# Attention set step by step between the matmul groups of two gated convolutions, on one core

## The chip, the cores and the metric

The kernel runs on one core of a Trainium2 chip. The metric is the time of one execution on the device, in microseconds (us). The time before is 488.39 us, the median of 3 runs (485.01 to 489.94).

## The reference

Three computations in a row. B = 4, H = 8 heads of 64 columns, S = 576, so the model width is 512.

```python
scores = (q @ k.T) / 8 + slope[h] * -abs(i - j)      # where 0 <= i - j < 128, else -1e9
attn = exp(scores - max(scores)); attn /= sum(attn) + 1e-9
x = attn @ v                                          # heads side by side: (4, 576, 512)

h = relu(x @ w_in)                                    # 1024 wide
g = h * sigmoid(conv3(h, taps1))                      # 3 taps along the sequence
x2 = g @ w_out                                        # 512 wide

gate = sigmoid(conv5(x2, taps2))                      # 5 taps, looking back
y = (gate * (x2 @ w_val)) @ w_out2
```

All is float32. The four weight products are made in three matmuls each, of tensors split in two parts (`hi` is the value rounded to fp32r, `lo` what is left): hi*hi, hi*lo, lo*hi.

## The kernel before, in words

Each engine has a program of its own, in a fixed order, and semaphores between them. There are two phases.

**Attention.** A step is one tile of 128 queries of one pair of heads: 4 batches x 4 pairs x 5 tiles = 80 steps; the fifth tile has 64 queries. Per step: TensorE makes the scores (`scores`, L743, a float32 matmul is two instructions in the trace, matmuls at L756); VectorE adds the bias and takes the maximum (`scores`, L567, L582); ScalarE makes the exp and its sum (`exps`, L401, L408); VectorE adds 1e-9 (`guard`, L596), inverts (`invert`, L605) and scales (`normalise`, L614); TensorE transposes (`turn`, L760, L777); ScalarE, for the fifth tile VectorE, copies the transposes out (`copy_out`, L422 and L626); TensorE multiplies by v (`mix`, L780, L805 and L808); ScalarE copies the result to `x_all` (`x_rows`, L430 and L433). The order is pair by pair, all five tiles of a pair. Scores run 5 steps ahead (`AHEAD`), with 5 buffers of probs, 2 banks each for scores, transposes and outputs. Meanwhile SyncE loads 12 weight panels (128 x 1024) into two raw buffers, one behind each pair's q and k, and GpSimd splits each: a cast to `w_hi` (L345) and a subtraction to `w_lo` (L348).

**Gated convolutions.** 8 chunks of 288 rows of the sequence, one half of a batch each. TensorE's order in a chunk c (`chunk`, L910): `up(c)` (8 groups of 12 matmuls of 290 columns), `val(c-1)` (4 groups), `down(c)` (4 groups of 24), `out(c-1)` (4 groups): 288 matmuls, all at L839 to L841 (in chunk 0 the first `down` is at L893 to L895). VectorE makes the taps of one block in the first convolution (`tap_rows`, L668 and L672), woven so that tap 0 of the next block stands between taps 1 and 2 of this one; then `gated` (L680), `val_rows` (L690), and five taps of the second convolution (`conv2_rows`, L702 and L706). ScalarE copies out of the banks, makes the sigmoids (L470, L493) and the `hi` parts (L479, L488, L511, and L450 for x), GpSimd the `lo` parts (L370, L362, L379, and L356 for x). `val_rows(0)` stands between the last two `gated`.

The loops over batches and chunks are loops on the engines (`Fori`).

Of the kernel before, what the change touches and what calls it, by code (L numbers as in the profile page):

```python
# [13 lines left out]
P = 128  # L14

# [5 lines left out]
SUBS = SEQ // SUB  # L25
SEEN = WINDOW + SUB
STEPS = PAIRS * TILES


AHEAD = 5  # L30
RING = TILES
SCALE = HEAD ** -0.5
MASKED = -1e9
# [3 lines left out]
EARLY = 16  # L37
# [27 lines left out]
def attention_and_gated_convolutions(nc, q_in, k_in, v_in, panels_in, taps1_in, taps2_in, y_out):  # L65
    with ExitStack() as ctx:
# [6 lines left out]


# [9 lines left out]

        w_hi = place("w_hi", [P, PANELS, PANEL], F32R)
        w_lo = place("w_lo", [P, PANELS, PANEL], F32R)
        x_all = place("x_all", [P, BATCH * PAIRS * SEQ])
        x_hi = place("x_hi", [P, KM, READ], F32R)
        x_lo = place("x_lo", [P, KM, READ], F32R)
        taps1 = place("taps1", [P, TAPS1, KW])  # L90
        taps2 = place("taps2", [P, TAPS2, KM])
        shared = top[0]


        q_heads = [place(f"q_heads{s}", [P, SUBS, 2, SUB]) for s in range(2)]
        k_pair = [place(f"k_pair{s}", [P, SEQ]) for s in range(2)]
        v_pair = [place(f"v_pair{s}", [P, TILES, P]) for s in range(2)]
        bias = place("bias", [P, PAIRS, SEEN])
        distance = place("distance", [P, SEEN])
# [7 lines left out]
        w_raw = [place(f"w_raw{r}", [P, PANEL]) for r in range(2)]  # L107


        top[0] = shared  # L110
        g1_hi = place("g1_hi", [P, KW, HALF], F32R)
        g1_lo = place("g1_lo", [P, KW, HALF], F32R)
        x2_all = place("x2_all", [P, KM, LEFT + SEQ])
# [7 lines left out]
        g2 = [place(f"g2_{r}", [P, HALF]) for r in range(2)]  # L121
        y_sb = [place(f"y_sb{r}", [P, HALF]) for r in range(2)]


        banks = [psum(f"bank{n}", [P, 512]) for n in range(8)]
        s_ps = [banks[0], banks[1]]
        t_ps = [banks[2], banks[3]]
        o_ps = [banks[4], banks[5]]
        o_tail_ps = banks[6]


        h_ps = x2_ps = banks[0:4]
# [829 lines left out]
```

## Time and profile before

| | before |
|---|---|
| median of 3 runs | 488.39 us |
| lowest and highest | 485.01, 489.94 us |
| profiled execution, span | 489.8 us |
| profiled execution, listed time nearest to the span | 489.94 us |
| instructions | 10856 |

The profile is one execution. PE is TensorE's matmuls, PEld its weight loads, DVE is VectorE, ACT is ScalarE, POOL is GpSimd, SP is SyncE, which issues the DMAs. The span goes from the first to the last instruction. Matmuls are pipelined, so a matmul's duration is longer than the time from one to the next. PEclk is the granted TensorE clock, 1.00 being 2.4 GHz and 0.50 being 1.2 GHz.

### The profile page before, as it was taken

The page shows a single profiled execution, that of the slowest core. Times are in us where ns is not written, and L with a number is a line of the kernel's source. Part 1 is how long each engine was busy: PE and PEld are TensorE (multiplying, and loading weights), DVE is VectorE, ACT ScalarE, POOL GpSimd, SP SyncE. Part 2 cuts the span into 40 slices and gives each one's busy share as a digit, 9 for nine tenths or more (in the row PEclk, how much of TensorE's full clock was granted, in tenths as well). Part 3 has the DMA queues.
Part 4 walks back from the last instruction along what each step waited for, and adds up shares of the span by engine and source line. Part 5 has one row for each costly group of instructions (what it writes and reads, how often), then busy time and mean ns, then how long its engine had stood idle before and what let it go on. Part 6 is the DMA issues. An engine that isn't in the chain of part 4 may idle for free.

```text
span 489.8 us, 10856 instructions
## 1 busy us (share of the span) xinstructions
PE 453.4 (93%) x3424; PEld 415.2 (85%) x3424; DVE 370.8 (76%) x1078; ACT 247.8 (51%) x746; POOL 177.9 (36%) x181
## 2 busy tenths in 40 slices
PE   4989788887889998999999999999999999999997
PEld 3767566665667897998999999999999999999996
DVE  5889967787767586896696786977968769669750
ACT  3777656775748563354354355255344344435432
POOL 2223522243310026157148136326425605713611
PEclk9999979998879998999999999999999999999999
DMA  5465435433413000000100000010010010010011
GB/s 146 116 176 149 148 106 168 154 115 115 141 49 98 1 2 0 2 1 1 50 1 1 32 17 0 12 36 0 0 48 0 0 48 0 0 48 2 1 48 50
DMA packets 37626, 25.52 MB, mean 52 GB/s; under 512 B 20704, under 2 KB 34016, under 8 KB 37600
## 3 DMA queue, kind: packets, MB, share of 16 engines
q1 hardware_dynamic: 37600, 25.20, 17.1%
q8 instruction: 14, 0.23, 0.2%
q14 instruction: 12, 0.10, 0.1%
HBM read 20.47 MB, written 4.72 MB: 51 GB/s over the span
## 4 chain that ended last, share of the span: by engine, by line
issue 33%; PE 28%; DVE 17%; POOL 16%; ACT 2%; DMA 1%; POOLq 1%; DVEq 0%; SPq 0%; ACTq 0%; PEldq 0%
POOL g_lo L370 10%; PE bank L756 7%; PE bank L777 7%; PE bank L808 5%; DVE guarded L596 4%; POOL x_lo L379 4%; DVE probs L614 3%; DVE conv L672 3%; PE bank L839 2%; PE bank L841 2%; PE bank L840 2%; POOL g_lo L362 2%; DVE gate L706 2%; DVE conv L680 1%; DVE probs L582 1%
## 5 line engine op out<-in xcount | busy, mean ns | idle before, releaser
L839 PE MATMUL bank<-x_hi,w_hi 128*128 128x290 f32 (+1 forms) x384 | 113.8, 296 | 0.5 <-ACT hidden L464 0.5
L840 PE MATMUL bank<-x_lo,w_hi 128*128 128x290 f32 (+1 forms) x384 | 113.7, 296 | 0.0
L841 PE MATMUL bank<-x_hi,w_lo 128*128 128x290 f32 (+1 forms) x384 | 113.7, 296 | 0.0
L839 PE MATMUL bank<-g_hi,w_hi 128*128 128x288 f32 x352 | 105.4, 300 | 3.2 <-POOL g_lo L370 1.7
L370 POOL TENSOR_TENSOR g_lo<-conv,g_hi 128x288 fp32r<-128x288 f32 x64 | 60.2, 949 | 131.2 <-ACT g_hi L479 131.2
L840 PE MATMUL bank<-g_lo,w_hi 128*128 128x288 f32 x352 | 103.9, 295 | 0.0
L841 PE MATMUL bank<-g_hi,w_lo 128*128 128x288 f32 x352 | 103.6, 294 | 0.0
L706 DVE SCALAR_TENSOR_TENSOR gate<-x_all,taps,gate 128x288 f32<-128x288 f32 x128 | 80.7, 630 | 4.5
L672 DVE SCALAR_TENSOR_TENSOR conv<-hidden,taps,conv 128x288 f32<-128x288 f32 x128 | 83.4, 657 | 0.6
L839 PEld LDWEIGHTS bank<-x_hi,w_hi 128*128 128x128 f32 x384 | 72.3, 188 | 0.8 <-ACT hidden L464 0.8
L840 PEld LDWEIGHTS bank<-x_lo,w_hi 128*128 128x128 f32 x384 | 72.8, 189 | 0.0
L841 PEld LDWEIGHTS bank<-x_hi,w_lo 128*128 128x128 f32 x384 | 72.5, 189 | 0.0
L408 ACT ACTIVATE probs<-probs,neg_max 128x192 f32<-128x192 f32 (+1 forms) x144 | 62.1, 434 | 20.2 <-DVE neg_max L582 19.2
L839 PEld LDWEIGHTS bank<-g_hi,w_hi 128*128 128x128 f32 x352 | 66.1, 188 | 6.8 <-POOL g_lo L370 5.7
L582 DVE CUSTOM_DVE_ANT_0 probs<-bank,bias 128x192 f32<-128x192 f32 (+1 forms) x144 | 46.5, 324 | 31.3 <-PE bank L756 22.0
L756 PE MATMUL bank<-k_pair,q_heads 128*128 128x192 f32 (+2 forms) x288 | 63.3, 345 | 6.9 <-DMA k_pair<-k_t 6.9
L777 PE MATMUL bank<-identity,probs 128*128 128x128 f32 x256 | 48.8, 306 | 20.4 <-DVE probs L614 20.2
L841 PEld LDWEIGHTS bank<-g_hi,w_lo 128*128 128x128 f32 x352 | 66.2, 188 | 0.0
L840 PEld LDWEIGHTS bank<-g_lo,w_hi 128*128 128x128 f32 x352 | 66.1, 188 | 0.0
L777 PEld LDWEIGHTS bank<-identity,probs 128*128 128x128 f32 x256 | 28.5, 149 | 35.2 <-DVE probs L614 24.1
L470 ACT ACTIVATE conv<-conv 128x288 f32<-128x288 f32 x64 | 28.5, 445 | 54.8 <-DVE conv L672 54.8
L756 PEld LDWEIGHTS bank<-k_pair,q_heads 128*128 128x128 f32 x288 | 49.4, 214 | 7.0 <-issue 6.8
(55 smaller groups left out, 670.8 us busy)
## 6 DMA issues: line engine op xcount, KB each, us to landing
w_raw<-panels SPq DMA_DIRECT2D x12, 512.0 KB, 4.2
q_heads<-q_t SPq DMA_DIRECT2D x32, 144.0 KB, 3.1
k_pair<-k_t SPq DMA_DIRECT2D x16, 288.0 KB, 3.7
y_t<-y_sb SPq DMA_DIRECT2D x32, 144.0 KB, 1.8
v_pair<-v_pairs SPq DMA_DIRECT2D x16, 256.0 KB, 2.7
v_pair<-v_pairs SPq DMA_DIRECT2D x16, 32.0 KB, 2.5
taps<-taps SPq DMA_DIRECT2D x1, 12.0 KB, 3.6
taps<-taps SPq DMA_DIRECT2D x1, 10.0 KB, 3.9
```

What stands on the lines that cost most here:

```text
L370: pool.tensor_tensor(g1_lo[:, m, :], conv[m % DEPTH][:, :], g1_hi[:, m, :], ALU.subtract).then_inc(g1_lo_done, 1)
L408: last = act.activation(probs[r][:, half, lo:hi], probs[r][:, half, lo:hi], ACT.Exp, bias=neg_max[r][:, half:half + 1], scale=-1.0, accum_ ...
L470: act.activation(conv[m % DEPTH][:, :], conv[m % DEPTH][:, :], ACT.Sigmoid).then_inc(gate1_done, 1)
L582: last = dve.tensor_tensor_reduce(probs[r][:, half, lo:hi], s[:, 2 * P * half + lo:2 * P * half + hi], bias_of(hp, t, half), -SCALE, 3e38, ...
L672: dve.scalar_tensor_tensor(out=out, in0=rows, scalar=taps1[:, tap, m:m + 1], in1=out, op0=ALU.mult, op1=ALU.add).then_inc(tap1_done if tap ...
L706: dve.scalar_tensor_tensor(out=out, in0=x2_all[:, m, at + tap:at + tap + HALF], scalar=taps2[:, tap, m:m + 1], in1=out, op0=ALU.mult, op1= ...
L756: last = pe.matmul(s[:, 2 * P * half + lo:2 * P * half + hi], q[:, 2 * t + half, :, :], k[:, first_key + lo:first_key + hi], start=True, s ...
L777: last = pe.transpose(out[:, at:at + P], p[:, half, col:col + P], identity[:, :])
L808: last = pe.matmul(o_ps[hp % 2][rows, t * P:(t + 1) * P], v[:, key_tile, rows], turned_probs, start=(j == 0), stop=(j == blocks - 1))
L839: pe.matmul(out, w_hi[:, p, col:col + P], hi[k], start=first, stop=False)
L840: pe.matmul(out, w_hi[:, p, col:col + P], lo[k], start=False, stop=False)
L841: last = pe.matmul(out, w_lo[:, p, col:col + P], hi[k], start=False, stop=final)
```

## The change

The program of each engine is written out in full over 9 x 24 beats, without loops. A beat of TensorE is one group of 12 matmuls. The attention steps go tile by tile over the four pairs of heads. Steps 0 to 11 (three tiles) run alone at the start; the others are set singly between beats: in even chunks c the steps 12 to 19 of the same batch before the beats 12 to 19 (`down`), in chunks 1, 3 and 5 the steps 0 to 11 of the next batch before the beats 10 to 21. Around each such beat TensorE runs `turn(step)` and `scores(step + 3)` before it and `mix(step)` behind it. Sigmoids stand in the beats 0 to 8.

Scores run 3 ahead with 4 buffers of probs; there is one bank for transposes and one for outputs, `mix` of a tile's first step waiting for `x_lo_done` of the tile before. x is no longer kept in float32: ScalarE casts the output bank to `x_hi` and VectorE subtracts to `x_lo`, per tile. Weight panels are loaded into the memory of `w_lo` and split in place; GpSimd splits six of them before the walk and six in chunk 0. All `copy_out` are ScalarE's. `hidden` and `conv` have 3 buffers instead of 4. The taps of a block are no longer woven with the next block's. q, k and v are laid out by tile on the host. Core of the diff:

```diff
-AHEAD = 5
-RING = TILES
+LOOK = 3
+RING = LOOK + 1
+V_RING = 3
+BEATS = 24
+VAL0, DOWN0, OUT0 = KW, KW + KM, BEATS - KM
-DEPTH = 4
+DEPTH = 3
...
+        def steps_before(c, j):
+            if c % 2 == 0 and c < CHUNKS and 0 <= j - DOWN0 < 8:
+                return [STEPS * (c // 2) + 12 + j - DOWN0]
+            if c % 2 == 1 and c < CHUNKS - 1 and 0 <= j - DOWN0 + 2 < 12:
+                return [STEPS * (c // 2 + 1) + j - DOWN0 + 2]
+            return []
+        def walk(slot, close, beat):
+            for step in range(12):
+                slot(step)
+                if step:
+                    close(step - 1)
+            close(11)
+            for c in range(CHUNKS + 1):
+                for j in range(BEATS):
+                    for step in steps_before(c, j):
+                        slot(step)
+                    beat(c, j)
+                    for step in steps_before(c, j):
+                        close(step)
...
# SyncE
+            load_queries_and_keys(0)
+            load_values(0)
+            load_panel(0)
+            load_queries_and_keys(1)
+            load_values(1)
+            sp.dma_start(taps1[:, :, :], taps1_in).then_inc(taps_loaded, 16)
+            sp.dma_start(taps2[:, :, :], taps2_in).then_inc(taps_loaded, 16)
+            load_panel(1)
+            load_panel(2)
...
# GpSimd
+            def beat(c, j):
+                if c < CHUNKS and 2 <= j < KW + 2:
+                    g1_low(c, j - 2)
+                if c > 0 and 0 <= j - VAL0 - 2 < KM:
+                    g2_low(c - 1, j - VAL0 - 2)
+                if c < CHUNKS and j == VAL0 + 3:
+                    keep_history(c)
+                if c < CHUNKS and j >= DOWN0 + 2 and j < DOWN0 + 2 + 2 * KM and j % 2 == 0:
+                    x2_low(c, (j - DOWN0 - 2) // 2)
+                if c == 0:
+                    for n in {3: (6,), 6: (7,), 14: (8, 9), 18: (10, 11)}.get(j, ()):
+                        split_panel(n)
+            for n in range(6):
+                split_panel(n)
+            walk(slot, slot, beat)
...
# ScalarE
+            def slot(step):
+                _, t, _ = where(step)
+                cols = 2 * P if t in (0, FULL) else 4 * P
+                act.wait_ge(turned, step + 1)
+                reach(act, mixed, step - 1)
+                act.copy(probs_t[step % 2][:, 0:cols], t_ps[:, 0:cols]).then_inc(copied, 1)
+                if step + LOOK - 1 < ALL_STEPS:
+                    exps(step + LOOK - 1)
...
+            def beat(c, j):
+                if c < CHUNKS and j < KW:
+                    hidden_rows(c, j)
+                if c < CHUNKS and 1 <= j < KW + 1:
+                    gate_rows(c, j - 1)
+                if c > 0 and j < KM:
+                    gate2_rows(c - 1, j)
+                if c < CHUNKS and 2 <= j < KW + 2:
+                    g1_high(c, j - 2)
+                if c > 0 and 0 <= j - VAL0 - 1 < KM:
+                    g2_high(c - 1, j - VAL0 - 1)
+                if c < CHUNKS and DOWN0 <= j < OUT0 and j % 2 == 1:
+                    x2_rows(c, (j - DOWN0) // 2)
+                if c > 0 and j >= OUT0:
+                    out_rows(c - 1, j - OUT0)
...
# VectorE
+            def slot(step):
+                if step + 1 < ALL_STEPS:
+                    normalise(step + 1)
+                if step + LOOK < ALL_STEPS:
+                    scores(step + LOOK)
...
+            def beat(c, j):
+                if c < CHUNKS and j < KW:
+                    tap_rows(c, j)
+                if c < CHUNKS and 1 <= j < KW + 1:
+                    gated(c, j - 1)
+                if c > 0 and 0 <= j - VAL0 < KM:
+                    val_rows(c - 1, j - VAL0)
+                if c < CHUNKS and DOWN0 + 2 <= j <= OUT0 and j % 2 == 0:
+                    conv2_rows(c, (j - DOWN0 - 2) // 2)
...
+            dve.wait_ge(taps_loaded, 32)
+            normalise(0)
+            walk(slot, close, beat)
...
# TensorE
+            def slot(step):
+                turn(step)
+                if step + LOOK < ALL_STEPS:
+                    scores(step + LOOK)
...
+            def beat(c, j):
+                if c < CHUNKS and j < VAL0:
+                    up(c, j)
+                if c > 0 and VAL0 <= j < DOWN0:
+                    val(c - 1, j - VAL0)
+                if c < CHUNKS and DOWN0 <= j < OUT0:
+                    down(c, (j - DOWN0) // 2, (j - DOWN0) % 2)
+                if c > 0 and j >= OUT0:
+                    out(c - 1, j - OUT0)
...
+            walk(slot, mix, beat)
```

`down(c, m, 0)` now waits for `g2_done` of the chunk before (its bank is the one `val` wrote), `out(c, 0)` for all four `g2_lo` of its chunk, `up(c, m)` for `y_kept` of the chunk c-2, and `up(c, 0)` for `x_lo_done` of the tiles it reads. On ScalarE and VectorE `close` of the last pair's step makes `x_hi` and `x_lo`; VectorE's `normalise` is now guard, invert and the two scalings in a row, each waiting for the one before.

## Rows read from the trace of the kernel before

**Rows 1.** The page: busy time of each engine, share of the span, instructions
```profile
PE 453.4 (93%) x3424; PEld 415.2 (85%) x3424; DVE 370.8 (76%) x1078; ACT 247.8 (51%) x746; POOL 177.9 (36%) x181
```
**Rows 2.** Stretches: its length, busy us (instructions) of each engine, clock, DMA share, GB/s
```profile
12.10:166.30 154.20, 134.02 (x1096) 101.46 (x1096) 121.34 (x591) 104.64 (x373) 43.49 (x25) 0.93 0.41 122
...
238.70:278.00 39.30, 39.16 (x293) 38.70 (x292) 30.89 (x58) 17.21 (x45) 16.99 (x17) 1.00 0.05 16
```
**Rows 3.** Timeline of TensorE, attention and both ends: start, us, what [idle before]
```profile
12.10 0.66 PE L777 MATMUL bank<-identity,probs 128*128 128x128 f32 x2 [0.22 <-DVE probs L614]
...
34.75 0.66 PE L777 MATMUL bank<-identity,probs 128*128 128x128 f32 x4 [1.22 <-DVE probs L614]
...
137.00 1.11 PE L777 MATMUL bank<-identity,probs 128*128 128x128 f32 x4 [3.48 <-DVE probs L614]
...
146.23 0.65 PE L777 MATMUL bank<-identity,probs 128*128 128x128 f32 x4
...
154.12 0.65 PE L777 MATMUL bank<-identity,probs 128*128 128x128 f32 x4
...
166.88 0.40 PE L839 MATMUL bank<-x_hi,w_hi 128*128 128x290 f32 x1
...
486.65 0.29 PE L841 MATMUL bank<-g_hi,w_lo 128*128 128x288 f32 x1
```
**Rows 4.** Timeline of TensorE in one chunk: first `up` and first `down` matmul
```profile
238.69 0.30 PE L839 MATMUL bank<-x_hi,w_hi 128*128 128x290 f32 x1
...
257.92 0.30 PE L839 MATMUL bank<-g_hi,w_hi 128*128 128x288 f32 x1
```
**Rows 5.** Timeline around one panel's split; then an undisturbed round of five steps
```profile
30.20 1.04 POOL L345 CAST w_hi<-w_raw 128x1024 f32 x1 [5.65 <-DMA w_raw<-panels]
...
30.38 1.20 DVE L614 TENSOR_SCALAR probs<-probs,inverse 128x192 f32<-128x192 f32 x2
...
31.41 2.39 POOL L348 TENSOR_TENSOR w_lo<-w_raw,w_hi 128x1024 f32 x1 [0.17 <-POOL w_hi L345]
31.51 2.32 DVE L596 TENSOR_SCALAR guarded<-total 128x2 f32<-128x2 f32 x1
...
34.16 0.54 DVE L614 TENSOR_SCALAR probs<-probs,inverse 128x192 f32<-128x192 f32 x2
...
146.23:154.12 7.89, 7.89 (x73) 6.05 (x71) 6.05 (x40) 6.59 (x26) 0.00 (x0) 1.00 0.42 112
```
**Rows 6.** The stretch behind the idle time that ends at 137.00
```profile
137.00:143.00 6.00, 6.00 (x28) 4.79 (x30) 2.02 (x17) 2.77 (x10) 0.00 (x0) 0.51 0.02 6
```
**Rows 7.** DMA issues: count, size of one, median us from issue to landing
```profile
w_raw<-panels SPq DMA_DIRECT2D x12, 512.0 KB, 4.2
```
**Rows 8.** Timeline of VectorE in the chunks
```profile
237.83 2.18 DVE L706 SCALAR_TENSOR_TENSOR gate<-x_all,taps,gate 128x288 f32<-128x288 f32 x4
...
250.03 0.51 DVE L672 SCALAR_TENSOR_TENSOR conv<-hidden,taps,conv 128x288 f32<-128x288 f32 x1
250.46 0.45 DVE L680 TENSOR_TENSOR conv<-hidden,conv 128x288 f32<-128x288 f32 x1
250.83 0.51 DVE L672 SCALAR_TENSOR_TENSOR conv<-hidden,taps,conv 128x288 f32<-128x288 f32 x1
...
251.54 1.06 DVE L672 SCALAR_TENSOR_TENSOR conv<-hidden,taps,conv 128x288 f32<-128x288 f32 x1
...
253.60 1.06 DVE L672 SCALAR_TENSOR_TENSOR conv<-hidden,taps,conv 128x288 f32<-128x288 f32 x1
...
270.58 0.36 DVE L702 TENSOR_SCALAR gate<-x_all,taps 128x288 f32<-128x288 f32 x1
...
273.50 0.37 DVE L702 TENSOR_SCALAR gate<-x_all,taps 128x288 f32<-128x288 f32 x1
```
**Rows 9.** Timeline of ScalarE: the first Sigmoid
```profile
172.45 1.28 ACT L470 ACT_TABLE_LOAD   x1
173.75 0.45 ACT L470 ACTIVATE conv<-conv 128x288 f32<-128x288 f32 x1
```

More of the change, by code:

```diff
@@ L453, in _ @@
-            for t in range(AHEAD - 1):
-                exps(0, 0, t)
-            copy_out(0, 0, 0)
-            batches(act, batch_tiles, lambda: split_x(0, 0, 0))
+            def slot(step):
+                _, t, _ = where(step)
+                cols = 2 * P if t in (0, FULL) else 4 * P
[4 more added lines that the diff above has]
+                    exps(step + LOOK - 1)
@@ L711, in chunk @@
[L711 to L729 removed]
+            for step in range(LOOK):
+                scores(step)
@@ L758, in scores, with turn @@
                 last.then_inc(scores_done, 1)
[L760 to L771 removed]
+            def turn(step):
+                _, t, _ = where(step)
+                pe.wait_ge(probs_normal, step + 1)
+                reach(pe, copied, step)
@@ L811, in mix @@
-                last.then_inc(mixed, 1)
-            def batch_tiles(b, last):
-                for hp in range(PAIRS):
-                    for t in range(TILES):
-                        ahead(b, hp, t, last, 1, turn)
-                        ahead(b, hp, t, last, AHEAD, scores)
-                        mix(b, hp, t)
+                        last = pe.matmul(o_ps[rows, P * hp:P * hp + SUB * subs],
+                                         v_tile[key_tile % V_RING][0:keys, P * hp + HEAD * h:P * hp + HEAD * (h + 1)],
+                                         turned_probs[0:keys, :, j, h, :], start=(j == 0),
+                                         stop=(j == blocks - 1))
@@ new lines, in mix, with slot, product @@
+                last.then_inc(mixed, 1)
+            def slot(step):
+                turn(step)
+                if step + LOOK < ALL_STEPS:
+                    scores(step + LOOK)
+            def product(out, w_at, hi, lo, of, first=True, final=True):
+                for i, k in enumerate(of):
+                    p, col = w_at(k)
+                    start, stop = first and i == 0, final and i == len(of) - 1
+                    pe.matmul(out, w_hi[:, p, col:col + P], hi(k), start=start, stop=False)
+                    pe.matmul(out, w_hi[:, p, col:col + P], lo(k), start=False, stop=False)
+                    last = pe.matmul(out, w_lo[:, p, col:col + P], hi(k), start=False, stop=stop)
+                return last
@@ L900, in out @@
-            def out(c):
-                ready = lambda k: since(pe, g2_lo_done, KM * c + k + 1)
-                for m in range(KM):
-                    since(pe, g2_done, KM * c + m + 1)
-                    product(y_ps[m % KM][:, 0:HALF], lambda k: (P_OUT2 + k // 2, k % 2 * MODEL + m * P),
-                            rows_of(g2_hi, KM), rows_of(g2_lo, KM),
-                            None if m else ready).then_inc(y_done, 1)
-            def chunk(c, batch, half):
-                up(c)
-                if is_chunk(c, 0):
-                    first_down()
-                    return
-                val(c - 1)
-                down(c)
-                out(c - 1)
@@ L921, in _ @@
-            since(pe, w_split, PANELS)
-            chunks(pe, chunk)
-            val(CHUNKS - 1)
-            out(CHUNKS - 1)
+            walk(slot, mix, beat)
 def kernel(**inputs):
```

759 lines of the change are left out of this document (290 added, 469 removed).

## The prediction

> **What bounds the kernel now.** I read the page's busy shares first [rows 1]: TensorE is busy 453.4 of 489.8 us, far above every other engine, so the question is whether the change takes anything out of its idle time. Then the stretches [rows 2] and TensorE's timeline. Attention runs from the first transpose at 12.10 us to the first matmul of `up` at 166.88; the gated convolutions from there to the last matmul at 486.65, which ends at 486.9 [rows 3]; the last copy and store take the 2.9 up to 489.8. TensorE's clock in attention is 0.93 on average and 1.00 in the chunk of [rows 2]. The matmul rows give what TensorE needs without waits. Five attention steps in a row, undisturbed, take 154.12 - 146.23 = 7.89 us, 1.58 a step [rows 3]. From the first `up` to the first `down` of a chunk, 144 matmuls take 257.92 - 238.69 = 19.23 us, 0.1335 each [rows 4]; the chunks need 8 x 288 of them, 307.6 us. So TensorE's own need is 12.1 + 80 x 1.58 less 1.9 for three scores already made = 124.5, + 307.6 + 2.9 = 447. Before loses 43 us over that: some 30 in attention, 12.4 in the chunks. In steady state a chunk takes 39.3 us [rows 2], TensorE 38.4 of them. The most that the change can win is 43 us, and only by less waiting: no matmul goes away, so two things that are both TensorE's own work can't hide each other.
>
> Where do the 30 us of attention come from? Each panel's split on GpSimd is a cast of 1.04 and a subtraction of 2.39 us [rows 5]. VectorE's `normalise` beside the cast takes 1.20 us for two where 0.54 is normal, its `guard`, two columns wide, 2.32 beside the subtraction (it starts 0.10 after GpSimd's row and ends with it; I take 0.15 as its own). So one panel takes 0.7 + 2.2 = 2.9 us from VectorE, which is busy for only 6.05 us of a round's 7.89 [rows 5]; TensorE loses what is left over that slack, 1.22 us of idle in [rows 3]. And after the longer idle of 3.48 us before 137.00 its granted clock is 0.51 on average over 6 us, so at the lower of its two levels, 1.2 GHz of 2.4, for nearly all of them [rows 3, 6]: that loses 2.9. I argue from these two prices throughout: 2.9 us of VectorE a panel, and half speed after a long wait.
>
> **What is removed, added, moved.**
> Work that stays: all matmuls, exps, taps and splits. The Tensor program gets a fixed order: slot (turn, scores three steps on), one group of 12 matmuls, mix. Fewer buffers: one bank for transposes, one for the output, 4 rings for probs instead of 5, 3 for conv instead of 4. At the edges: `copy_out` of the last tile moves from VectorE to ScalarE (16 copies), x_lo from GpSimd to VectorE (20 times, 512 columns mostly; from the 0.45 of 288 columns [rows 8] I estimate 0.7 each, 14 us). TensorE's order doesn't feel these by themselves.
>
> Start. `normalise(0)` now waits for the taps, which are queued behind panel 0, q, k and v of tile 1. Before, the first transpose is at 12.10 [rows 3], with the same q and k ahead of it; a panel more in the queue is 4.2 us to landing [rows 7]. I let it stand at 12.1 (bounds 11 and 16).
>
> Prologue, 12 steps alone. TensorE needs 12 x 1.58 = 19.0 less the scores already made, so 17.0 and an end at 29.1. But six panels are now split in these first 30 us, where before GpSimd paused 5.65 us between two [rows 5]. Now it hardly pauses: a panel lands within 4.2 us [rows 7], 3.6 us of splitting follow, so about three are back to back. A step has three VectorE instructions that such a split stops (guard, two normalise) and a panel offers two boundaries, so while GpSimd works back to back I take one step per 3.5 us instead of 1.6 to 1.9. From 13 us: three panels, 11 us, 3 steps; then two more with gaps, 11 us, 4.5 steps; the other 4.5 steps at 1.9, 9 us; the first x tile's way bank, ScalarE, VectorE before the first `up` costs 2 us that no TensorE work covers. End: about 43. Bounds: 32 (VectorE's slack of 0.3 us a step takes up most of it) and 50. I take 43 since panel and step prices are rows. 14 us over need.
>
> Chunk 0. TensorE needs 192 x 0.1335 + 8 x 1.58 = 38.2. VectorE: a block of taps took 2.06 us in before's order (253.60 - 251.54), of which 0.55 is GpSimd's subtraction (the 1.06 where 0.51 is normal) [rows 8]. In the new order the three taps of a block follow each other, each waiting for the last; such a pair costs 0.55 (2.18 us for four, the last 0.51 long) where an unchained one costs 0.43 (250.46 - 250.03) and `gated` 0.37 (250.83 - 250.46) [rows 8]; tap 0 I take at 0.40. So 0.40 + 0.55 + 0.43 + 0.37 + 0.55 = 2.3 us a block, 18.4 for eight. A conv2 block is 2.92 us (273.50 - 270.58) [rows 8], four are 11.7. Attention steps: I take 6.05/5 = 1.21, plus 0.1 for chaining; eight are 10.5, two x tiles 1.4. Together 42, and now six panels on top, 6 x 2.9 = 17, of which the last 5 run on into the next chunk: 54, with some of it before and behind. Its first mix stands behind ScalarE's g1_high(7), which waits for all eight blocks and two panels, 25 us in, when TensorE is there at 16. I take 49 us (bounds 40 and 58), 11 over need.
>
> Chunks 1, 3, 5 (12 steps each). Need 288 x 0.1335 + 12 x 1.58 = 57.4. VectorE needs 18.4 + 4 x 0.4 + 12 x 1.31 + 3 x 0.7 + 11.7 = 49.5, so it isn't the bound of the sum. But it falls behind at the front: the taps start 2.4 us in (a group of 1.6, then copy and waits, estimated 0.8) and with the wait for the last sigmoid the last `gated` ends at 21.7; `val_rows(0)` and ScalarE's g1_high(7), g2_high(0) end at 22.6. ScalarE's queue holds the copy of the first interleaved step behind them: 23.2. TensorE wants that copy, for `mix` after beat 10, at 11 x 1.6 for the beats and 1.3 for one turn and scores (my share of 1.58 to 1.9), 18.9. Wait: 4.3 us. The low clock behind such a wait I price at 2.6 us, a little under the 2.9 of [rows 3, 6] (bounds 0, where a wait of 1.22 lowered nothing, and 2.9). 57.4 + 4.3 + 2.6 = 64.3, taken as 64.4. From there VectorE has 2.9 + 2 x 1.31 + 0.4 = 5.9 us of work for two beats of 2 x (1.6 + 1.58) = 6.4, so nothing further is lost. Chunk 1 takes over VectorE's lag from the late panels: 66.5.
>
> Chunks 2, 4, 6 (8 steps). Need 51.0. Here the slot comes before beat 12, `down`'s first part wants `g2_done` at 22.1 and TensorE is there at 12 x 1.6 + 1.2 = 20.4; the copy behind it is late by 0.3. 53.4. Chunk 7, without steps: there at 19.2, so 2.9 of wait and 0.7 of clock: 42.0, against 39.3 now: the early `val_rows(0)` and the taps woven into each other are what before saves. Tail: val and out 12.8, the chain from the last `val` to a now undivided wait for four g2_lo 2.1, end 2.9: 17.8.
>
> ScalarE: Exp and Sigmoid now alternate by chunk, 14 loads where there were two, 1.28 us each with the Sigmoid starting 1.30 after the load's start [rows 9]. ScalarE is busy 17.2 of 39.3 us [rows 2], so 14 x 1.28 = 18 us mostly fit in. The first exp of a set is needed two slots (6.8 us) later: cost nothing, up to 1.3 a set if the lag above eats it. The Trainium skill (ScalarE: Activation LUTs, What ACT_TABLE_LOAD costs) puts a switch at about 2.66 us, since a drain of 1.38 comes with it. Our row shows no such gap. By the page the loads would be 37 us of ScalarE; 1.4 more in each of 7 sets is the most that can reach TensorE, 10 us.
>
> The unrolled program is fetched instead of looped over; no row prices that, 0 to 5 us; I take 0.
>
> Sum: 43 + 49 + 66.5 + 2 x 64.4 + 3 x 53.4 + 42 + 17.8 = 507.3 against the span of 489.8. The listed time nearest this span is 489.94, so nothing lies around it; the median of the three is 488.39, 1.4 lower. Predicted: **506 us**.
>
> **Rivals.**
> (a) Faster. VectorE keeps step: if the eight tap blocks end by 18.9 us of a chunk (2.0 us a block rather than 2.3, gate and copy right behind), no wait at the first mix arises, and no low clock. Then chunks 1 to 7 lose nothing: 447 + 14 + 11 + 2 = 474. For it: before's own blocks take 2.06 [rows 8]. Against: three waits in a row per block and the in-order queue on ScalarE.
> (b) No change. The panels cost half: VectorE works between them, as in the round of [rows 3, 5] where a panel costs TensorE 1.22 us, and prologue and chunk 0 end at 36 and 43: 507 - 13 - 5 (no lag, less clock) = 489, 488 by the median.
> (c) Much slower. The slot's loop (copy, exp, normalise, turn, each behind another engine's queue) also stalls in each beat with conv2: 1 us for 16 such pairs and the clock at half more often: 525.
> (d) By the switch price of the drain: some 516. It asks for a gap of 1.4 us behind the table load, which the one row of a load amid work does not show.
>
> **How the numbers follow.** Forecast 0.55, (a) 0.13, (b) 0.12, (c) 0.14, (d) 0.06. The prologue's bounds alone are 32 and 50, chunk 0's 40 and 58. The range reaches into (a) and (c): 478 to 530. About 1% is what a measurement of this kernel can tell from no change. Faster by over 1% holds (a) and the low edge of the forecast, 0.15; within 1% (b), 0.13; slower the rest, 0.72.
>
> **What would show it.** Right: TensorE idle before the first `mix` of the odd chunks, 3 to 5 us, with ScalarE's copy of probs_t as what it waits for, and the clock at 0.5 behind it; the first `up` at 40 us or later; VectorE's guard and normalise at 2.3 us several times in the first 40 us; chunk 0 the only chunk with GpSimd busy over 30 us; 14 to 16 table loads. Wrong: a first `up` before 35, or chunks 3 and 5 under 60 us; a fall of TensorE's idle time below 30 us in all.

## The result, and the profile after

The changed kernel takes 512.43 us (median of 4 runs, 510.67 to 514.14), the kernel before 488.97 beside it: a ratio of 1.048, 95% interval 1.0415 to 1.0546. It is slower. The profiled execution took 511.86 us for a span of 509.9. The page of the changed kernel, busy time, and the chain that ended last by engine:

```profile
PE 453.4 (89%) x3424; PEld 421.6 (83%) x3424; DVE 382.4 (75%) x1080; ACT 259.9 (51%) x756; POOL 152.8 (30%) x178
...
PE 53%; DVE 33%; issue 6%; ACT 5%; SPq 1%; DMA 1%; POOLq 0%; POOL 0%; DVEq 0%
```

TensorE is busy for the same 453.4 us as in [rows 1], so the 20 us of added span show as TensorE's idle time. (The busy time holds what a lower clock costs; the mean clock is 0.956 here and 0.976 before.) The losses lie in few places. Stretches of the changed kernel from one first matmul of `up` to the next (columns as in [rows 2]): the 12 steps at the start, chunks 0 to 4, chunk 7, the tail.

```profile
13.80:45.35 31.55, 23.55 (x168) 17.79 (x169) 28.29 (x98) 17.97 (x63) 17.10 (x10) 0.95 0.58 188
45.35:106.98 61.63, 41.73 (x304) 38.40 (x304) 50.78 (x102) 24.26 (x68) 31.89 (x25) 0.83 0.14 41
106.98:172.04 65.06, 61.45 (x457) 57.32 (x457) 51.00 (x160) 36.17 (x108) 13.55 (x17) 0.95 0.12 34
172.04:222.84 50.80, 50.28 (x403) 47.38 (x401) 39.42 (x110) 28.11 (x80) 13.38 (x17) 1.00 0.15 42
222.84:287.11 64.27, 60.88 (x458) 56.48 (x457) 48.74 (x155) 36.57 (x109) 13.56 (x17) 0.95 0.16 43
287.11:337.90 50.79, 50.27 (x402) 47.36 (x401) 39.35 (x110) 28.12 (x80) 13.38 (x17) 1.00 0.15 41
450.82:490.62 39.80, 38.56 (x291) 38.33 (x289) 30.11 (x56) 17.60 (x45) 13.47 (x17) 1.00 0.05 16
490.62:509.90 19.28, 14.74 (x98) 14.27 (x96) 1.83 (x4) 5.07 (x13) 3.21 (x4) 0.90 0.13 45
```

Even chunks (172.04, 287.11) lose half a microsecond. The start loses 8 (31.55 less 23.55), chunk 0 loses 20 and ran at clock 0.83, odd chunks lose 3.5 and part of their clock. TensorE's waits by what ended them (total us, times, longest):

```profile
PE bank L621 <- DVE probs L512: 17.9, 14, 4.8
PE bank L642 <- ACT probs_t L387: 17.7, 4, 8.9
PE bank L658 <- DVE x_lo L527: 6.6, 2, 5.1
PE bank L607 <- DMA k_all<-k_t: 5.9, 1, 5.9
```

The first is `turn` waiting for `normalise`: 11.3 of it up to the first `up`, 4.8 of these before the first transpose, and 4.0 once in chunk 0. The second is the predicted wait: the first interleaved `mix` of chunks 0, 1, 3 and 5. Here is the one of chunk 3, 21.4 us into it, the timeline and then the clock (columns of a stretch as above):

```profile
243.37 0.43 ACT L427 CAST g_hi<-gate 128x288 fp32r<-128x288 f32 x1
243.71 0.37 ACT L387 COPY probs_t<-bank 128x256 f32<-128x256 f32 x1
244.09 1.28 ACT L376 ACT_TABLE_LOAD   x1
...
244.22 0.70 PE L642 MATMUL bank<-probs_t,v_tile 128*64 128x128 f32 x4 [2.96 <-ACT probs_t L387]
...
245.39 0.35 ACT L376 ACTIVATE probs<-probs,neg_max 128x64 f32<-128x64 f32 x1
```
```profile
245.00:247.00 2.00, 1.65 (x7) 1.66 (x7) 1.70 (x9) 1.99 (x9) 0.60 (x2) 0.50 0.00 0
247.00:249.00 2.00, 2.00 (x9) 2.00 (x9) 1.21 (x6) 0.86 (x5) 1.35 (x3) 0.50 0.00 0
```

The copy stands in ScalarE's queue right behind g2_high, as forecast, TensorE waits 2.96 us for it, and then runs at 0.50, 1.2 GHz.

In chunk 0 the panels are added. Timeline of GpSimd and VectorE at panel 6, TensorE's first `mix` and a later `turn`, and GpSimd and VectorE at the last panel but one:

```profile
56.51 2.49 POOL L320 TENSOR_TENSOR w_lo<-w_raw,w_hi 128x1024 fp32r<-128x1024 f32 x1
56.66 2.51 DVE L538 TENSOR_SCALAR conv<-hidden,taps 128x288 f32<-128x288 f32 x1
58.95 0.86 POOL L326 TENSOR_TENSOR g_lo<-conv,g_hi 128x288 fp32r<-128x288 f32 x1
...
72.18 1.12 PE L642 MATMUL bank<-probs_t,v_tile 128*64 128x128 f32 x8 [8.92 <-ACT probs_t L387]
...
87.85 0.69 PE L621 MATMUL bank<-identity,probs 128*128 128x128 f32 x2 [3.95 <-DVE probs L512]
...
98.11 2.36 POOL L320 TENSOR_TENSOR w_lo<-w_raw,w_hi 128x1024 fp32r<-128x1024 f32 x1
98.23 7.25 DVE L570 SCALAR_TENSOR_TENSOR gate<-x_all,taps,gate 128x288 f32<-128x288 f32 x4
```

A tap that takes 0.36 us elsewhere took 2.51, and four taps of the second convolution, beside two panels, took 7.25 where [rows 8] show 2.18. The latter stand ahead of the next tile's `x_lo`, for which `up` of chunk 1 waited 5.1 us. The `turn` at 87.85 waited behind the panels 8 and 9 in the same way. The 8.92 us before the `mix` are another matter: chunk 0 has no `val` beats, so TensorE is there 17.9 us into the chunk, and ScalarE's copy, behind `g1_high(7)`, comes at 26.8. Only 0.8 us of it goes when GpSimd's subtractions go (8.08 left in experiment 5).

### The profile page after: what moved, and what is told of

The parts are those of the page before. It is cut to its first block, busy times and chain, and to the rows that moved or that the text cites. A ratio compares the mean times of both kernels' runs of the same rounds, so it can differ in the third digit from the quotient of the medians.

```text
span 509.9 us, 9587 instructions
## 1 busy us (share of the span) xinstructions
PE 453.4 (89%) x3424; PEld 421.6 (83%) x3424; DVE 382.4 (75%) x1080; ACT 259.9 (51%) x756; POOL 152.8 (30%) x178
## 4 chain that ended last, share of the span: by engine, by line
PE 53%; DVE 33%; issue 6%; ACT 5%; SPq 1%; DMA 1%; POOLq 0%; POOL 0%; DVEq 0%
DVE conv L543 13%; PE bank L658 11%; PE bank L659 11%; PE bank L660 11%; PE bank L607 7%; PE bank L621 7%; PE bank L642 6%; DVE conv L550 5%; DVE conv L538 4%; DVE gate L570 3%; DVE probs L512 2%; DVE guarded L505 2%; ACT L431 2%; DVE gate L557 2%; DMA taps<-taps 1%
## 5 line engine op out<-in xcount | busy, mean ns | idle before, releaser
L658 PE MATMUL bank<-g_hi,w_hi 128*128 128x288 f32 x384 | 123.6, 322 | 5.5 <-POOL g_lo L326 1.9
L659 PE MATMUL bank<-g_lo,w_hi 128*128 128x288 f32 x384 | 114.8, 299 | 0.0
L660 PE MATMUL bank<-g_hi,w_lo 128*128 128x288 f32 x384 | 114.8, 299 | 0.0
L387 ACT COPY probs_t<-bank 128x512 f32<-128x512 f32 (+1 forms) x80 | 40.1, 502 | 83.4 <-PE bank L621 83.4
L658 PEld LDWEIGHTS bank<-g_hi,w_hi 128*128 128x128 f32 x384 | 73.9, 192 | 7.8 <-DVE gate L557 2.9
L607 PE MATMUL bank<-k_all,q_tile 128*128 128x192 f32 (+2 forms) x288 | 62.6, 341 | 5.9 <-DMA k_all<-k_t 5.9
L336 POOL TENSOR_TENSOR x_lo<-x_all,x_hi 128x288 fp32r<-128x288 f32 x32 | 26.4, 826 | 134.5 <-ACT x_hi L441 134.5
L642 PE MATMUL bank<-probs_t,v_tile 128*64 128x128 f32 (+2 forms) x576 | 49.7, 285 | 17.7 <-ACT probs_t L387 17.7
L376 ACT ACTIVATE probs<-probs,neg_max 128x192 f32<-128x192 f32 (+2 forms) x144 | 62.1, 435 | 5.8 <-DVE neg_max L494 5.7
L621 PE MATMUL bank<-identity,probs 128*128 128x128 f32 x256 | 47.9, 302 | 18.2 <-DVE probs L512 17.9
L512 DVE TENSOR_SCALAR probs<-probs,inverse 128x192 f32<-128x192 f32 (+2 forms) x144 | 58.3, 442 | 2.8
```

Of the source, the lines that this page charges most:

```text
L376: last = act.activation(probs[r][:, half, lo:hi], probs[r][:, half, lo:hi], ACT.Exp, bias=neg_max[r][:, half:half + 1], scale=-1.0, accum_ ...
L387: act.copy(probs_t[step % 2][:, 0:cols], t_ps[:, 0:cols]).then_inc(copied, 1)
L512: last = dve.tensor_scalar(probs[r][:, half, lo:hi], probs[r][:, half, lo:hi], inverse[r][:, half:half + 1], None, ALU.mult)
L607: last = pe.matmul(s_ps[step % 2][:, 2 * P * half + lo:2 * P * half + hi], q_tile[tile % 2][:, hp, half, :, :], k_all[:, hp, first_key + l ...
L621: last = pe.transpose(t_ps[:, at:at + P], probs[step % RING][:, half, col:col + P], identity[:, :])
L642: last = pe.matmul(o_ps[rows, P * hp:P * hp + SUB * subs], v_tile[key_tile % V_RING][0:keys, P * hp + HEAD * h:P * hp + HEAD * (h + 1)], t ...
```

## The experiments

The table sums up where time lay: the first matmul of the first `up`, then the chunks' lengths from one first `up` to the next, and the tail, all from the profiled execution of each kernel.

| | first up | c0 | c1 | c2 | c3 | c7 | tail |
|---|---|---|---|---|---|---|---|
| forecast | 43 | 49 | 66.5 | 53.4 | 64.4 | 42.0 | 17.8 |
| changed kernel | 45.35 | 61.6 | 65.1 | 50.8 | 64.3 | 39.8 | 19.3 |
| a_split_dve | 42.6 | 50.2 | 63.7 | 50.8 | 63.2 | 39.8 | 17.8 |
| a_late | 47.2 | 51.9 | 70.0 | 50.9 | 63.5 | 39.8 | 19.3 |
| a_shift | 46.0 | 61.6 | 62.6 | 51.0 | 61.1 | 39.8 | 19.3 |
| a_one_table | 46.4 | 61.2 | 64.2 | 50.4 | 64.0 | 39.3 | 17.8 |
| a_two | 45.1 | 50.6 | 61.2 | 50.9 | 61.1 | 39.8 | 17.8 |
| a_woven | 45.9 | 64.7 | 68.6 | 54.4 | 67.8 | 43.1 | 17.8 |
| a_woven4 | 44.9 | 62.9 | 67.7 | 52.8 | 66.4 | 41.5 | 17.8 |

In the table a_split_dve is experiment 1, a_late 2, a_shift 3, a_one_table 4, a_two 5, a_woven 7 and a_woven4 8. Unless said otherwise an experiment is the changed kernel with one edit, and its ratio is to the kernel before.

**1. The panels' subtraction on VectorE.** In the changed kernel; the calls stand in VectorE's slots 1, 2, 3, 6, 9, 11 and in chunk 0's beats 2, 5, 13, 15, 17, 19, and GpSimd's casts go to the beats 2, 5, 12, 15.

```diff
 # GpSimd, split_panel
-                pool.wait_ge(w_rounded, n + 1)
-                pool.tensor_tensor(w_lo[:, n, :], w_raw[:, n, :], w_hi[:, n, :],
-                                   ALU.subtract).then_inc(w_split, 1)
 # VectorE
+            def panel_low(n):
+                dve.wait_ge(w_rounded, n + 1)
+                dve.tensor_tensor(w_lo[:, n, :], w_raw[:, n, :], w_hi[:, n, :],
+                                  ALU.subtract).then_inc(w_split, 1)
```

> The changed kernel, but each panel's subtraction (12 of them) is made by VectorE instead of GpSimd; the cast stays on GpSimd. Theory (GpSimd's subtraction locks VectorE out, and the panels are bunched in the prologue and chunk 0): a subtraction costs VectorE about 1.2 us instead of 2.2 of lockout, and the boundaries go; first `up` from 45.4 to 38 or earlier, chunk 0 from 61.6 to 50 or less, the later chunks within 1 us: 490 to 495 us in all. Rival (the step loop itself, with 3 steps of lead and single banks, sets prologue and chunk 0): VectorE only gets more work, first `up` and chunk 0 within 3 us of what they are, 508 to 515.

Measured: 499.66 us (494.05 to 500.59), ratio 1.021 (1.0108 to 1.0312), 12.8 less than the changed kernel, where 490 to 495 was expected. The same subtraction, by groups of instructions with count, total and mean ns, is dearer on GpSimd (the changed kernel) than on VectorE (this one):

```profile
L320 POOL TENSOR_TENSOR w_lo<-w_raw,w_hi 128x1024 fp32r<-128x1024 f32 x12 | 28.9, 2409 | 1.0
```
```profile
L515 DVE TENSOR_TENSOR w_lo<-w_raw,w_hi 128x1024 fp32r<-128x1024 f32 x12 | 15.4, 1283 | 0.0
```

So VectorE does in 1.28 us what, done by GpSimd, stopped it for 2.2. Chunk 0 went from 61.6 to 50.2. But the start went only to 42.6, and that in the fastest execution (494.05); experiment 5 has the same start and its first `up` at 45.1. So moving the subtraction, which still costs VectorE 1.28 us a panel, brought the start 0.2 to 2.8 us. What the panels cost there as a whole is asked in experiment 6.

**2. The panels 8 to 11 in chunk 1.**

```diff
-                    for n in {3: (6,), 6: (7,), 14: (8, 9), 18: (10, 11)}.get(j, ()):
+                    for n in {3: (6,), 6: (7,)}.get(j, ()):
+                        split_panel(n)
+                if c == 1:
+                    for n in {2: (8,), 5: (9,), 13: (10,), 17: (11,)}.get(j, ()):
```

> The changed kernel, but the panels 8 to 11 are split in chunk 1 (one each at the beats 2, 5, 13, 17) instead of in chunk 0 (two each at 14 and 18). Theory (VectorE's lockout by two panels back to back binds chunk 0): chunk 0 from 61.6 to 49 to 52, chunk 1 from 65 to 69 to 72, 506 in all. Rival (chunk 0 is bound by the order of the steps): chunk 0 stays above 58, chunk 1 grows, 512 or more.

Measured: 506.09 us (503.13 to 508.54), ratio 1.031 (1.0199 to 1.0421). Chunk 0 got 9.7 us shorter, chunk 1 4.9 longer. The two numbers aren't the same loss at two places. In chunk 0 the first `mix` waits 8.91 us as before, so the four panels have no part in that wait. In chunk 1 the first `val` waits for the panels 8 and 9 themselves (GpSimd's row of panel 9, then TensorE's):

```profile
117.79 2.43 POOL L320 TENSOR_TENSOR w_lo<-w_raw,w_hi 128x1024 fp32r<-128x1024 f32 x1
...
120.32 0.58 PE L661 MATMUL bank<-x_hi,w_hi 128*128 128x288 f32 x1 [8.16 <-issue]
```

What the four would cost in chunk 1 by holding VectorE alone, this run doesn't show.

**3. The steps of the odd chunks two beats later.**

```diff
-            if c % 2 == 1 and c < CHUNKS - 1 and 0 <= j - DOWN0 + 2 < 12:
-                return [STEPS * (c // 2 + 1) + j - DOWN0 + 2]
+            if c % 2 == 1 and c < CHUNKS - 1 and 0 <= j - DOWN0 < 12:
+                return [STEPS * (c // 2 + 1) + j - DOWN0]
```

> The changed kernel, but in chunks 1, 3 and 5 the twelve steps stand before the beats 12 to 23 instead of 10 to 21. Theory (in the odd chunks TensorE waits at the first mix, since ScalarE's copy is queued behind the g_hi casts of blocks that VectorE finishes late, and then runs at half clock): by beat 12 the copy is no longer late by more than 1 us, so of the 7 us over need 5 to 6 go, and about 2 come back where the next chunk's `up` now waits for x_lo: chunks 3 and 5 at 59 to 61.5 us instead of 64, some 9 less in all, 503. Rival (VectorE's or ScalarE's sum in the odd chunks is what binds): odd chunks stay at 64 or grow, 510 or more.

Measured: 504.27 us (502.64 to 505.2), ratio 1.0282 (1.0177 to 1.0387), chunk 3 at 61.1. The stretch that ran at 0.50 in the changed kernel shows the full clock here:

```profile
245.00:247.00 2.00, 2.00 (x16) 1.92 (x14) 1.60 (x7) 1.61 (x8) 1.03 (x2) 1.00 0.13 38
```

Chunk 3 gained 3.2 us, but its wait and clock were more than that, since the shift brings other waits. The whole chunk in the shifted kernel:

```profile
221.19:282.25 61.06, 58.59 (x459) 54.23 (x457) 47.65 (x155) 37.02 (x110) 13.39 (x17) 1.00 0.19 49
```

TensorE is busy for 58.6 us at full clock and waits 2.5: 0.5 before `down`, 0.5 before a `turn`, and 1.4 before the next chunk's `up`, for `x_lo`. In the changed kernel chunk 3 had 3.4 us of waits and was busy for 60.9, so 2.3 us more for the clock; the prediction had 4.3 and 2.6.

**4. One table.** Both Sigmoids become Exp, so this kernel computes other gates; the instructions are otherwise the same and one table load is left of 16.

```diff
-ACT.Sigmoid
+ACT.Exp
```

> The changed kernel with both Sigmoids replaced by Exp, so the values differ from the reference but ScalarE loads its table once instead of 16 times. Theory (a switch is 1.28 us and is mostly covered): at most 1.3 us in each of the seven sets of steps, likely 0 to 4 us in all, 508 to 512. Rival (a switch costs its drain too, 2.7 us, and is on the path of every set): 10 to 18 us less, 495 to 502.

Measured: 508.22 us (508.07 to 509.15), ratio 1.038 (1.0276 to 1.0484). Fifteen loads fewer bring some 4 us, and 1.5 of them are the tail's clock. In the rows at 244.09 and 245.39 above a load takes 1.28 and the exp begins 1.30 after its start.

**5. Both remedies of 1 and 3.**

> The changed kernel with the panels' subtraction on VectorE and the odd chunks' steps from beat 12 on, and nothing else. Theory (the two losses are separate and add: 499.66 with the first alone, 8 us less by the second alone): 489 to 494, chunk 0 at 50, chunks 3 and 5 at 61. With them gone the changed order stands about where the kernel before does, since 12 steps at the start and VectorE's 42 us of work in chunk 0 stay as they are. Rival (the wait moved on to a later beat only seemed gone since GpSimd set the pace elsewhere): 496 or more.

Measured: 490.42 us (488.39 to 493.1, 10 runs), ratio 1.0034 (0.9988 to 1.008), no difference from the kernel before. The two gains add: 512.4 - 12.8 - 8.2 = 491.5. They are as large as the slowdown, but the kernel before still pays for GpSimd's subtractions, which this one doesn't; experiment 11 makes the like comparison. The first `mix` of chunk 0 still waits:

```profile
70.30 1.12 PE L649 MATMUL bank<-probs_t,v_tile 128*64 128x128 f32 x8 [8.08 <-ACT probs_t L384]
```

**6. No panel beside the 12 steps.** GpSimd waits for all 12 before it splits anything.

```diff
+            pool.wait_ge(mixed, 12)
             for n in range(6):
                 split_panel(n)
```

> The changed kernel, but GpSimd begins with the panels only when the twelve steps of the prologue are done. This is a look at the prologue without panels; the time as a whole is not what is asked, since `up` of chunk 0 now waits for four panels (some 14 us) behind the prologue. Theory (the panels hold VectorE and stretch the prologue): from the first transpose the steps follow every 1.6 to 1.9 us, the last mix ends at 34 to 36 instead of 43. Rival (the loop turn, copy, exp, normalise with three steps of lead binds, as VectorE's subtraction instead of GpSimd's gained only 2.8 us): 2.2 us a step or more, the last mix at 39 or later.

Measured, one execution: 522.32 us, span 520.3; the last `mix` of the start ends at 37.5, between the two theories (in the changed kernel at 43.9). TensorE's timeline, three `turn` of a full tile, and the last `mix`:

```profile
27.23 0.66 PE L622 MATMUL bank<-identity,probs 128*128 128x128 f32 x4
...
29.06 0.66 PE L622 MATMUL bank<-identity,probs 128*128 128x128 f32 x4
...
30.89 0.66 PE L622 MATMUL bank<-identity,probs 128*128 128x128 f32 x4
...
36.40 1.09 PE L643 MATMUL bank<-probs_t,v_tile 128*64 128x128 f32 x16
```

With nothing in the way a step of a full tile takes 1.83 us, without idle time. The 1.58 that I used is the average of a pair's five tiles [rows 3], two of which are cheaper; the 12 steps are tiles 0, 1 and 2. From the first transpose at 13.97 to 37.5 they take 23.5 us, 1.4 of them idle, where I had 17.0. The step time is the theory's, the end is later than it said.

**7. Taps woven again.** VectorE's order per block is tap 1, tap 0 of the next block, tap 2, `gated`, as before the change.

```diff
-                if c < CHUNKS and j < KW:
-                    tap_rows(c, j)
+                if c < CHUNKS and j < KW:
+                    if j == 0:
+                        tap_rows(c, 0, 0)
+                    tap_rows(c, j, 1)
+                    if j + 1 < KW:
+                        tap_rows(c, j + 1, 0)
+                    tap_rows(c, j, 2)
```

> The changed kernel with the taps woven as before the change: tap 0 of the next block between taps 1 and 2 of this one. Theory (a tap chained to the one in front costs 0.12 us more; the eight blocks of a chunk end late for the first mix or for `down`): a block 2.06 instead of 2.18 us, the eighth block 1.0 us earlier, which each of the chunks 0 to 7 gives on to TensorE where it waits for it: 4 to 8 us less, 504 to 508. Rival (weaving doesn't reach TensorE): 511 to 514.

Measured: 539.32 us (538.01 to 539.8), ratio 1.1019 (1.0937 to 1.1102): 27 us slower than the changed kernel, a plain miss. The timeline of VectorE, GpSimd and ScalarE shows why:

```profile
242.77 0.37 DVE L538 TENSOR_SCALAR conv<-hidden,taps 128x288 f32<-128x288 f32 x1 [1.32 <-POOL g_lo L326]
...
243.60 0.44 ACT L413 ACTIVATE conv<-conv 128x288 f32<-128x288 f32 x1 [1.50 <-DVE conv L543]
...
244.29 0.42 ACT L421 CAST g_hi<-conv 128x288 fp32r<-128x288 f32 x1
...
244.78 0.81 POOL L326 TENSOR_TENSOR g_lo<-conv,g_hi 128x288 fp32r<-128x288 f32 x1 [2.12 <-ACT g_hi L421]
...
245.69 0.37 DVE L538 TENSOR_SCALAR conv<-hidden,taps 128x288 f32<-128x288 f32 x1 [1.33 <-POOL g_lo L326]
```

Tap 0 of block m+1 writes a `conv` buffer that g_lo of block m-2 must have read; that g_lo waits for ScalarE's g_hi, which stands in ScalarE's queue behind a sigmoid, which waits for a tap of VectorE. It is a loop over three engines, 2.92 us a block. Unwoven, tap 0 comes one block later and the loop is slack: the changed kernel's blocks take 2.18.

**8. A fourth buffer for `conv`**, laid over the last quarter of `g2_lo`, otherwise as 7.

```diff
+        conv.append(nc.alloc_sbuf_tensor_at("conv3", [P, HALF], F32,
+                                            offset=base + g2_lo_at + 4 * HALF * (KM - 1)))
...
-                    reach(dve, g1_lo_done, n - DEPTH + 1)
+                    reach(dve, g1_lo_done, n - CRING + 1)
```

> The changed kernel with the taps woven and a fourth buffer for conv (laid over the last quarter of g2_lo, which is free in beats 0 to 12); all else as in a_woven. Theory (the ring of three is what made weaving dear): in a_woven tap 0 of the next block waited for GpSimd's g_lo of the block three back, which stands behind the sigmoid that waits for VectorE's last tap, a loop of 2.92 us a block (245.69 - 242.77). With four buffers the wait goes one block further back and a block falls to 2.1 or less: odd chunks 62 to 64.5, even ones 50.8, chunk 7 39.8, in all 503 to 512 instead of 539. Rival (weaving itself is dear here, since VectorE stands before tap 0 of the next block until TensorE has made its group): blocks stay at 2.6 or more, 525 or more.

Measured: 527.37 us (526.7 to 529.17), ratio 1.0892 (1.0791 to 1.0993): 12 of the 27 us come back. The theory's time is missed; the time is the rival's, though a block takes 2.32 us and not the rival's 2.6. Another wait now ends last before tap 0:

```profile
241.69 0.70 DVE L544 TENSOR_SCALAR conv<-hidden,taps 128x288 f32<-128x288 f32 x1 [0.38 <-ACT hidden L413]
...
242.86 0.45 ACT L419 ACTIVATE conv<-conv 128x288 f32<-128x288 f32 x1 [1.20 <-DVE conv L549]
...
243.57 0.41 ACT L413 ACTIVATE hidden<-bank 128x290 f32<-128x290 f32 x1
...
244.01 0.71 DVE L544 TENSOR_SCALAR conv<-hidden,taps 128x288 f32<-128x288 f32 x1 [0.39 <-ACT hidden L413]
```

ScalarE's queue puts the copy `hidden` of block m+1 behind the sigmoid of block m-1, and that sigmoid waits for VectorE: 2.32 us a block (244.01 - 241.69). I take it that the weave needs ScalarE's copies to run further ahead as well; no run shows it.

**9. Everything together**, the remedies 1, 3 and 7 and the taps loaded before panel 0 (a_all), and the same with 8 (a_all4).

```diff
             load_values(0)
+            sp.dma_start(taps1[:, :, :], taps1_in).then_inc(taps_loaded, 16)
+            sp.dma_start(taps2[:, :, :], taps2_in).then_inc(taps_loaded, 16)
             load_panel(0)
```

> The changed kernel with four edits together: panels' subtraction on VectorE, the steps of the odd chunks two beats later, woven taps, and the taps loaded ahead of panel 0. Theory (the causes are separate and add up): 512 - 13 (subtraction) - 8 (two beats later) - 5 (woven) - 1 (taps load) = 485, 482 to 489. Rival (they are one wait, counted twice): 493 to 500.

> The changed kernel with the four remedies together: panels' subtraction on VectorE, odd chunks' steps from beat 12 on, taps woven with four conv buffers, taps loaded before panel 0. Theory (the losses are separate: 12 us by the subtraction, 8 by the late copy at the first mix, and the rest small): 484 to 492, first up at 41 to 43, chunk 0 at 50, odd chunks 61, even ones 51. Rival (one takes the other's place, or a block of taps stays above 2.6 us): 500 or more.

Measured: 516.66 us (514.02 to 516.77), ratio 1.0547 (1.0464 to 1.063), and 503.9 (502.22 to 506.37), ratio 1.0384 (1.0281 to 1.0487). Both expectations are missed. Both times are close to experiment 5's plus the weave's price (490.4 + 26.9 and 490.4 + 14.9). In a_all4 the first transpose is at 10.09 instead of 13.77, and yet the first `up` is at 44.67, so nearly nothing of it is left.

**10. The kernel before, with the subtraction on VectorE.** GpSimd keeps the cast; `panel_low` stands before step 1 of the pairs 1, 2 and 3 and the last step of pair 3 of each batch.

```diff
             def batch_tiles(b, last):
                 for hp in range(PAIRS):
                     for t in range(TILES):
+                        if not last and t == 1 and hp >= 1:
+                            panel_low(PAIRS * b + hp - 1, (hp - 1) % 2)
+                        if not last and t == 4 and hp == 3:
+                            panel_low(PAIRS * b + 3, 1)
```

> The kernel before the change, but each panel's subtraction is made by VectorE, one round of five steps after its load. Theory (in the kernel before, some 26 of its 30 us of attention waits are GpSimd's subtraction locking VectorE out, and the low clock behind): VectorE needs 6.05 + 1.2 us of a round's 7.9, which fits beside TensorE, so attention ends at 142 to 150 instead of 166.9, 465 to 475 us in all. Rival (VectorE's added 1.2 us and a new wait for the cast in its own queue cost as much): 484 to 492.

Measured: 481.37 us (478.56 to 484.33), ratio 0.985 (0.976 to 0.994); attention ends at 155.17 instead of 166.88. That is less than expected. TensorE's wait of 14.4 us in all is mostly three waits, one for each batch's last panel. The third, in the timeline:

```profile
119.22 1.04 POOL L344 CAST w_hi<-w_raw 128x1024 f32 x1 [7.72 <-DMA w_raw<-panels]
...
120.42 1.23 DVE L628 TENSOR_TENSOR w_lo<-w_raw,w_hi 128x1024 f32 x1 [2.52 <-POOL w_hi L344]
...
120.72 3.21 POOL L352 TENSOR_TENSOR x_lo<-x_all,x_hi 128x1160 fp32r<-128x1160 f32 x1 [0.46 <-ACT x_hi L446]
121.56 2.71 DVE L611 TENSOR_SCALAR probs<-probs,inverse 128x192 f32<-128x192 f32 x2
...
124.33 0.90 PE L783 MATMUL bank<-identity,probs 128*128 128x128 f32 x3 [5.52 <-DVE probs L611]
```

VectorE stood 2.52 us before a panel that wasn't there yet.

**11. The same, with that panel taken later.** VectorE's loop over batches is written out.

```diff
+                        n = PAIRS * b + hp - 1
+                        if t == 1 and 0 <= n < PANELS:
+                            panel_low(n, n % 2)
...
-            batches(dve, batch_tiles)
+            for b in range(BATCH):
+                batch_tiles(b, b == BATCH - 1)
```

> The kernel before with the panels' subtraction on VectorE, the fourth panel of a batch taken not at the batch's last step but at the second step of the next batch (the panels 0 to 11 at step 1 of the pairs 1 to 16). Theory (what b_split_dve has left is VectorE standing before a panel that isn't there yet, at 48.41, 86.07 and 124.33, 3.43 + 2.39 + 5.52 us of TensorE's idle time, each with half clock behind it, some 2.6): all three go, 19 us less at most, of which I expect 11 to 17: 464 to 471, attention's end at 138 to 145 instead of 155.17. Rival (these waits belong to the change of batch, where q and k come late, whatever the panels do): 478 to 482, waits of over 2 us at the same three places.

Measured: 468.53 us (468.0 to 469.33), ratio 0.9665 (0.9578 to 0.9753). It beats both kernels: its slowest execution is faster than any of theirs. Attention ends at 143.82. TensorE's waits in attention, before the change 20.2 us in 15 by the same view, are now

```profile
PE bank L783 <- DVE probs L611: 5.0, 11, 2.3
```

and the clock is 0.99 from the first transpose to the first `up`, where it was 0.93 [rows 2].

This gives the like comparison, both with the subtraction on VectorE: 490.42 us reordered (experiment 5), 468.53 in the old order. The pages, the reordered kernel (span 488.3) first:

```profile
PE 444.2 (91%) x3424; PEld 412.9 (85%) x3424; DVE 371.4 (76%) x1092; ACT 260.0 (53%) x756; POOL 126.5 (26%) x166
...
PE 445.8 (95%) x3424; PEld 409.3 (88%) x3424; DVE 361.6 (77%) x1090; ACT 246.4 (53%) x746; POOL 150.5 (32%) x169
```

TensorE is idle for 44 us in the one and 21 in the other (span 467.0). So the change, its order and its fewer buffers together, costs 22 us when neither side has GpSimd's subtractions, and these aren't the reason why it doesn't win. In the reordered kernel 11 us of the idle time lie before the first transpose, 8 in the start, 10 in chunk 0.

## Why the prediction was right, and where it wasn't

It said 506 us, slower; it is 512.43. The mechanism held: VectorE and the engines behind it are late, and TensorE waits and slows its clock. The number alone doesn't say so, since 512.43 lies 6 us above the forecast and 4 below rival (d)'s 516; experiment 4 and the chunks do.

**Right.** Chunks 1 and 3 at 66.5 and 64.4 came at 65.1 and 64.3, with the named wait on ScalarE's copy; the first `up` at 43 came at 45.35; 16 table loads of 1.28 us, at some 4 us of the whole time (forecast 0) for 15 of them; GpSimd over 30 us in chunk 0 alone (31.89). Rival (d), 10 us and a gap of 1.4 us behind the load, falls. The Trainium skill (ScalarE: Activation LUTs, What ACT_TABLE_LOAD costs) puts a switch at about 2.66 us, by which 15 loads would be an estimated 40 us of ScalarE. The trace doesn't agree: the exp begins 1.30 us after the load's start. One sign came only in part: VectorE's `guard` took 2.23 us once in the first 40 us and 1.60 to 1.76 three times, not 2.3 several times. Rival (a) falls with the odd chunks' wait, (b) with chunk 0. Rival (c), waits in the later beats with conv2, shows in chunk 0 only; even chunks lose 0.5 us.

**The term that was mis-sized: chunk 0, 49 us, measured 61.6.** TensorE's need is 38.2, so 23.4 us are lost where I had 11. The wait at the first `mix` was right: forecast 25 against 16 us, 9; measured 8.92. I had 54 us of VectorE work and let the last 5 run on into chunk 1, at no price here. They can't run on for nothing: the taps that the panels 8 to 11 hold stand ahead of a `normalise` and of the next tile's `x_lo`, and TensorE waits 3.95 and 5.1 us for these, and 1.9 before a matmul of `down`. The other 3.5 are the clock, 0.83 over the chunk (41.7 busy against 38.2). The price of a panel, 2.9 us of VectorE, was about right (2.51 on a 0.36 us tap beside the subtraction). With the subtraction moved, chunk 0 takes 50.2, and with the four panels out of it (experiment 2) 51.9.

**Right for a wrong reason: the start.** I had 12.1, then 17.0 of steps, 12 for panels, 2 for the handover. (The prediction's own count from 13 us, 11 + 11 + 9 + 2, comes to 46 and not to the 43 that it took.) Experiment 6 shows 13.97, then 23.5 of steps with no panel at all, to 37.5. The changed kernel's last `mix` ends at 43.9, so six panels cost 6.4 us, about half of my 12, and the steps 6.5 more; the handover is 1.4. The first transpose is late since `guard` waited 3.3 us for the taps. That these errors nearly cancel is luck.

**The odd chunks, term by term.** Of chunk 3's 64.3 us, 58.6 are TensorE's own time at full clock, 3.4 waits and 2.3 the clock (experiment 3); I had 57.4, 4.3 and 2.6. So mechanism and sizes held. A block of taps took 2.18 (2.3 forecast), which goes with the shorter wait. The need was 1.2 us more, since 1.58 a step is an average over five unlike tiles: tiles 0 to 2 take (58.6 - 38.4) / 12 = 1.68 between beats, tiles 3 and 4 (50.3 - 38.4) / 8 = 1.49. The same twelve steps kept TensorE busy for 22.1 us when they stood alone in experiment 6, against 20.2 between beats.

**The later even chunks and chunk 7.** Chunks 2 and 4 came 2.6 each and chunk 7 2.2 under the forecast, chunk 6 (49.7 us) 3.7: of the small waits I gave them 0.5 us is there in an even chunk and 1.2 in chunk 7. These 11.1 us make up for most of chunk 0's 12.6, so the total is nearer than its parts, by luck.

**The tail**, 19.3 against 17.8: the same wait as forecast, with the clock low behind it, and 2.0 us lie around the span where I had nothing.

## What to carry to other kernels

A large GpSimd operation beside a busy VectorE is priced by what it stops there, not by GpSimd's idle time: doing the subtraction on VectorE itself, placed where its input is surely there, took 20 us off the kernel before, where the reordering added 23. When a change is tried on a kernel with such a loss, take the loss out of both sides before judging the change. Before taking an order from one kernel to another, follow each ring of buffers round all its engines: a loop of three engines through three buffers set the pace of the weave. Work that is left over at the end of a stage isn't free if something that the next stage needs stands behind it in the same queue. An average step time holds only for the mix of tiles over which it was taken.

## What the hardware showed that I hadn't expected

The low clock isn't a fixed price of a wait. In the tails of the changed kernel and of a_two TensorE waits the same 1.88 us before the same matmul, and the stretches behind it (columns as above) differ, the changed kernel first:

```profile
499.00:504.00 5.00, 4.94 (x25) 4.94 (x26) 0.00 (x0) 0.40 (x1) 0.01 (x1) 0.66 0.09 30
```
```profile
478.90:483.90 5.00, 4.98 (x37) 4.98 (x38) 0.00 (x0) 0.80 (x2) 0.00 (x0) 1.00 0.13 45
```

One runs at 0.66 and one at 1.00. This is worth 1.5 us, and no run settles what decides it.

GpSimd's larger `x_lo`, 1160 columns and 3.21 us long in experiment 10, held VectorE as a panel does: two scalings beside it took 2.71 us where 0.54 is normal [rows 5].
